# Expert 0's transposed x: built on TensorE with 0/1 choices instead of scattered and read back

## What is computed

```python
# attention: q, k, v of (2, 8, 576, 64)
scores = scale * q @ k.T
kth    = the 32nd largest score of each row
scores = where(scores >= kth, scores, -1e9)
x      = softmax(scores) @ v            # then (1152, 512): one row per token

# mixture of 8 experts with one choice per token, at most 288 tokens each
logits = x @ w_gate
e      = argmax(logits);  gate_w = softmax(logits)[e]
pos    = how many earlier tokens chose the same expert
disp[e, pos] = x                        # if pos < 288, else dropped
y      = relu(disp @ w1[e]) @ w2[e]
x      = gate_w * y[e, pos]             # 0 for a dropped token

# a last layer
h = x @ w_in                            # 2048 wide
g = (a0 + a1 h + a2 h^2 + a3 h^3) / (1 + |b0||h| + |b1| h^2 + 1e-6)
out = g @ w_out
```

## Time and profile before

| what | us |
|---|---|
| median of 3 runs | 807.46 (806.16 to 808.84) |
| the profiled execution | 809.16 |
| its span, first to last instruction | 807.4 |
| PE busy | 740.2 (92%) |
| DVE busy | 658.3 (82%) |
| ACT busy | 491.8 (61%) |
| POOL busy | 359.7 (45%) |
| mean granted PE clock | 0.958 |

### The profile page before, as it was taken

The page is one execution under the profiler, slowest core; times in us unless marked ns, Lnnn a source line. Parts: engine busy times, 40 slices in busy tenths (PEclk is TensorE's granted clock), DMA queues, the critical chain, the costliest instruction groups (busy, mean ns, idle before and its releaser), DMA issues.

```text
span 807.4 us, 15534 instructions
## 1 busy us (share of the span) xinstructions
PE 740.2 (92%) x5370; PEld 692.8 (86%) x5370; DVE 658.3 (82%) x1664; ACT 491.8 (61%) x890; POOL 359.7 (45%) x531
## 2 busy tenths in 40 slices
PE   4899999999999999838999999999469999999997
PEld 4788899898898888728999999999469899898996
DVE  3999999999999999825767667675749988898885
ACT  6677676666677775434445444544547767767673
POOL 4646565545568784240000000000149678667764
PEclk9799999999999999967999999999769999999999
DMA  9640000600000202031657677586811002000001
GB/s 190 159 163 14 1 16 1 222 15 2 14 2 15 106 7 100 1 144 44 219 173 237 194 207 238 170 210 190 230 48 31 1 1 80 1 0 19 22 1 39
DMA packets 61978, 71.20 MB, mean 88 GB/s; under 512 B 21969, under 2 KB 41937, under 8 KB 61906
## 3 DMA queue, kind: packets, MB, share of 16 engines
q1 hardware_dynamic: 60466, 65.57, 27.5%
q0 software_dynamic: 1440, 4.72, 1.7%
HBM read 56.12 MB, written 14.16 MB: 87 GB/s over the span
## 4 chain that ended last, share of the span: by engine, by line
PE 58%; DVE 26%; DMA 5%; issue 4%; ACT 3%; POOL 2%; SPq 1%; DVEq 0%; ACTq 0%; POOLq 0%
PE bank L1400 16%; PE bank L1401 16%; PE bank L1402 16%; DVE best L739 8%; DVE pairs L741 5%; DVE best L760 3%; PE bank L1306 3%; DVE pairs L758 2%; PE bank L1282 2%; PE bank L1272 2%; DMA slots_out<-y_blocks 2%; DVE pairs L722 2%; DMA slot_rows<-slots_in 2%; DVE joined L769 1%; DVE least_kept L778 1%
## 5 line engine op out<-in xcount | busy, mean ns | idle before, releaser
L957 DVE RECIPROCAL r<-c 128x384 f32<-128x384 f32 x48 | 122.5, 2552 | 25.3 <-POOL c L678 25.2
L739 DVE MAX8 best<-pairs 128x8 f32<-128x288 f32 x288 | 130.9, 547 | 0.0
L1028 ACT ACTIVATE probsT<-bank 96x768 f32<-96x768 f32 x72 | 58.2, 808 | 95.5 <-PE bank L1289 95.5
L667 POOL DMA_INDIRECT x_rows<-slots_out,slot_index x9 | 11.2, 1240 | 225.8 <-DMA slots_out<-y_blocks 224.3
L1306 PE MATMUL bank<-v_rows,probsT 96*128 96x65 f32 (+1 forms) x960 | 106.5, 264 | 3.6 <-ACT probsT L1028 3.4
L741 DVE MATCH_REPLACE8 pairs<-best,pairs 128x288 f32<-128x288 f32 x216 | 109.7, 547 | 0.0
L1306 PEld LDWEIGHTS bank<-v_rows,probsT 96*128 96x128 f32 (+1 forms) x960 | 102.3, 181 | 8.0 <-ACT probsT L1028 6.8
L886 DVE TENSOR_TENSOR wl<-raw,wh 128x1024 fp32r<-128x1024 f32 x72 | 87.2, 1218 | 19.6 <-ACT wh L1122 19.2
L1136 ACT ACTIVATE hTh<-bank 128x288 fp32r<-128x288 f32 x64 | 26.5, 414 | 104.4 <-PE bank L1402 104.4
L1400 PE MATMUL bank<-xTh,wh 128*128 128x288 f32 x256 | 76.7, 300 | 12.9 <-DVE xTl L898 12.9
L577 POOL TENSOR_TENSOR pairs<-scores 128x288 int32<-128x288 int32 x72 | 57.7, 801 | 66.3 <-ACT scores L1014 65.9
(11 more groups left out here) (138 smaller groups left out, 2201.6 us busy)
## 6 DMA issues: line engine op xcount, KB each, us to landing
raw<-in_moe_w SPq DMA_DIRECT2D x16, 2048.0 KB, 8.9
slots_in<-zeros SPq DMA_DIRECT2D x18, 256.0 KB
slot_rows<-slots_in SPq DMA_DIRECT2D x32, 144.0 KB, 8.7
slots_out<-y_blocks SPq DMA_DIRECT2D x32, 144.0 KB, 8.2
raw<-in_moe_w_in SPq DMA_DIRECT2D x8, 512.0 KB, 8.0
v_rows<-in_v SPq DMA_DIRECT2D x16, 144.0 KB, 4.0
out_rows<-out_rows SPq DMA_DIRECT2D x9, 256.0 KB, 2.4
q_rows<-in_q SPq DMA_DIRECT2D x8, 256.0 KB, 3.1
```

Source lines behind the costliest of these rows:

```text
L739: ins = nc.vector.max(best, cur)
L957: nc.vector.reciprocal(rS[x][:], cS[x][:]).then_inc(s_d2, 1)
L1028: nc.scalar.activation(pT[x % 2][:], T_ps[0:KP, 0:KJ * P], ACT.Exp, scale=SCALE).then_inc(s_ex, 1)
```

## The change

Expert 0 gets its transposed x from PE. For each tile t, DVE makes `chosen[t]`, a 128x288 matrix of 0 and 1: row = token of the tile, column = slot of expert 0, 1 where the token has that slot (`choice`). x times gate weight is written as a high part by ACT (`x_high_part`) and a low part by DVE (`low`); PE sums x_hi[t]^T chosen[t] + x_lo[t]^T chosen[t] over the nine tiles in four banks, one for each 128 columns of x (`first_x`): 72 products in all. ACT and DVE take xTh and xTl of expert 0 out of these banks. The other experts still go through DRAM: all nine tiles are scattered, and now POOL itself multiplies x by the gate weight in place before each scatter (`gated`). The read and the turn of expert 0's rows are gone. w1[0] is loaded in four DMAs in the permuted order.

Beside that: the last head is turned in banks 0 and 1 (`turned`), so its turn doesn't wait for the exponential of the head before; `times_v` of the last three heads comes after both turns. The counts of earlier tokens of a whole tile are summed by DVE in three shifted additions (`oh2`, `oh4`, `ohb`), and PE needs two products where it had eight. The routing of tile 8 reads its logits straight from the bank.

The core of the diff, PE, POOL, SP and ACT:

```diff
+        def turned(x):
+            return S_ps if x == NH - 1 else T_ps
...
-            sp.wait_ge(s_sd, 16 * NT)
-            load_rows(0)
+            sp.wait_ge(s_sd[0], 16 * FIRST_OUT)
+            sp.wait_ge(s_sd[1], 16 * (NT - FIRST_OUT))
             def expert(e, first, last):
                 if not last:
-                    sp.wait_ge(s_xt, (e + 1) * DC)
+                    if not first:
+                        sp.wait_ge(s_xt, e * DC)
                     load_rows(e + 1)
...
+            def gated(t):
+                pool.wait_ge(s_xi, t + 1)
+                pool.wait_ge(s_xo, X0_ORDER.index(t) + 1)
+                x_ = xa[:, t * DM:(t + 1) * DM]
+                nc.gpsimd.tensor_scalar(x_, x_, gw[:, t:t + 1], None, ALU.mult).then_inc(s_xg, 1)
             for i, tiles in enumerate(GATED):
                 pool.wait_ge(s_ix, i + 1)
                 for t in tiles:
+                    gated(t)
                     pool.wait_ge(s_xg, t + 1)
                     nc.gpsimd.indirect_dma_start(
...
-            for i in range(NH + 1):
+            for i in range(NH):
                 slot(i)
+            short_of(NH - 2)
+            short_of(NH - 1)
             gate_exp(0)
-            slot(NH + 1)
-            gated(0)
+            exps(NH - 2)
+            exps(NH - 1)
+            act.wait_ge(s_gw, 1)
+            for t in range(LAST - 1):
+                x_high_part(t)
             x_turned(LAST)
-            logits_out(LAST)
+            x_high_part(LAST - 1)
             gate_exp(1)
-            gated(1)
+            act.wait_ge(s_gw, 2)
+            x_high_part(LAST)
...
+                    if first and f == 0:
+                        act.wait_ge(s_sd[0], 16 * FIRST_OUT)
                     nc.scalar.activation(hTh[f % 2][:], bank(f % 2)[:, 0:CAP], ACT.Relu).then_inc(s_hh, 1)
...
+            def first_x(t, ds):
+                n_ = min((t + 1) * P, CAP) if t else CAP
+                pe.wait_ge(s_ch, CHOICES.index(t) + 1)
+                for part in range(2):
+                    if part == 0:
+                        pe.wait_ge(s_xi, t + 1)
+                    else:
+                        pe.wait_ge(s_xo, X0_ORDER.index(t) + 1)
+                    for d in ds:
+                        if t == X0_ORDER[0] and part == 0 and d >= 2:
+                            pe.wait_ge(s_xn, LAST + d - 1)
+                        ends = t == X0_ORDER[-1] and part == 1
+                        last = nc.tensor.matmul(bank(X0_BANK[d])[:, 0:n_], (x_hi, x_lo)[part][t][:, d * P:(d + 1) * P],
+                                                chosen[t][:, 0:n_], start=(t == X0_ORDER[0] and part == 0), stop=ends)
...
-            for i in range(NH + 2):
+            for i in range(NH):
                 slot(i)
+            for x in (NH - 2, NH - 1):
+                turn_scores(x)
+                less_max(x)
+                drop(x)
             tokens_before_most()
-            times_v(NH - 1)
+            for x in (NH - 3, NH - 2, NH - 1):
+                times_v(x)
+            first_x(0, range(DC - 1))
             turn_x(LAST)
+            first_x(0, range(DC - 1, DC))
+            first_x(1, range(DC))
             logits(LAST)
+            for t in X0_ORDER[2:4]:
+                first_x(t, range(DC))
             tokens_before_last()
+            for t in X0_ORDER[4:]:
+                first_x(t, range(DC))
```

and DVE after the one-hots of tiles 0 to 7:

```diff
+            def choice(t):
+                if t == 0:
+                    dve.wait_ge(s_no, 1)
+                nc.vector.tensor_scalar(chosen[t][:], slot_no[:], c0[:, t:t + 1], oh[:, t * E:t * E + 1].bitcast(F32),
+                                        ALU.is_equal, ALU.mult).then_inc(s_ch, 1)
+            def low(t):
+                dve.wait_ge(s_xi, t + 1)
+                nc.vector.scalar_tensor_tensor(x_lo[t][:], xa[:, t * DM:(t + 1) * DM], gw[:, t:t + 1],
+                                               x_hi[t][:].bitcast(F32), ALU.mult, ALU.subtract).then_inc(s_xo, 1)
...
+            gate_weights(0)
+            last_x(0)
+            before_in_first(0)
+            slot_numbers(0)
+            for t in range(3):
+                choice(t)
+                low(t)
+            last_x(1)
+            for t in (3, 4):
+                choice(t)
+                low(t)
...
+            choice(5)
+            low(5)
+            gate_weights(1)
+            before_in_first(1)
+            choice(LAST)
+            choice(6)
+            low(6)
+            low(LAST)
+            choice(7)
+            low(7)
+            slot_numbers(1)
```

More of the change, by code:

```diff
@@ L812, in link @@
                 dve.wait_ge(s_gc, chain[0])
[L814 to L852, removed]
             def last_x(half):
@@ L870, in last_x, with by_e @@
                 ins.then_inc(s_xn, 1)
[L872 to L880, removed]
+            def by_e(t, part):
+                lo, n_ = GATED[part][0], len(GATED[part])
+                return t[:, lo * E:(lo + n_) * E].rearrange("p (t e) -> p t e", t=n_)
@@ new lines, in _ @@
+            dve.wait_ge(s_sum0, 3)
+            dve.wait_ge(s_oh, 1)
+            W = LAST * E
+            link(nc.vector.tensor_tensor(oh2[:, 2 * E:2 * E + W], ohz[:, E:E + W].bitcast(F32), ohz[:, 0:W].bitcast(F32), ALU.add))
+            link(nc.vector.tensor_tensor(oh4[:, 5 * E:5 * E + W], oh2[:, 2 * E:2 * E + W], oh2[:, 0:W], ALU.add))
+            with nc.allow_low_precision("counts are whole numbers"):
+                nc.vector.tensor_tensor(ohb[:], oh4[:, 4 * E:4 * E + NT * E], oh4[:, 0:NT * E], ALU.add).then_inc(s_os, 1)
@@ L901, in _ @@
             for d in range(DC):
-                x_turned(0, d)
-            for d in range(DC):
-                x_low(0, 0, d)
+                dve.wait_ge(s_xh, d + 1)
+                nc.vector.tensor_tensor(xTl[0][:, d, :], bank(X0_BANK[d])[:, 0:CAP], xTh[0][:, d, :].bitcast(F32),
+                                        ALU.subtract).then_inc(s_xl, 1)
+            dve.wait_ge(s_ab, 32)
+            nc.vector.tensor_scalar(ab[:, 6:8], ab[:, 4:6], -1.0, None, ALU.mult).then_inc(s_ab, 1)
+            dve.wait_ge(s_ab, 33)
+            nc.vector.tensor_tensor(ab[:, 6:8], ab[:, 6:8], ab[:, 4:6], ALU.max).then_inc(s_ab, 1)
             def y_out(e):
@@ L1095, in _, with x_high_part @@
             k_out(3, 1)
[L1096 to L1101, removed]
+            def x_high_part(t):
+                if t == LAST:
+                    act.wait_ge(s_fx, 1)
+                nc.scalar.activation(x_hi[t][:], xa[:, t * DM:(t + 1) * DM], ACT.Copy, scale=gw[:, t:t + 1]).then_inc(s_xi, 1)
             def gate_exp(part):
@@ L1288, in drop @@
                 for j in range(KJ):
-                    last = nc.tensor.matmul(T_ps[0:KP, j * P:(j + 1) * P], so[x % 2][:, j * KP:(j + 1) * KP], minus_big[:],
+                    last = nc.tensor.matmul(turned(x)[0:KP, j * P:(j + 1) * P], so[x % 2][:, j * KP:(j + 1) * KP], minus_big[:],
                                             start=False, stop=(j in (3, KJ - 1)), skip_group_check=True)
@@ L1329, in tokens_before_most @@
             def tokens_before_most():
-                pe.wait_ge(s_oh, 1)
+                pe.wait_ge(s_os, 1)
                 pe.wait_ge(s_const, 4)
[L1333 to L1339, removed]
@@ L1346, in tokens_before_last @@
                 pe.wait_ge(s_oh, 2)
[L1347 to L1348 removed]
+                nc.tensor.matmul(bank(COUNTS)[:, LAST * E:NT * E], tri[:], oh[:, LAST * E:NT * E], start=False, stop=True,
+                                 skip_group_check=True).then_inc(s_po, 1)
+            def first_x(t, ds):
[12 more added lines that the diff above has]
+                                                chosen[t][:, 0:n_], start=(t == X0_ORDER[0] and part == 0), stop=ends)
+                        if ends:
+                            last.then_inc(s_x0, 1)
+                if t == 0 and DC - 1 in ds:
+                    last.then_inc(s_fx, 1)
```

114 lines of the change are left out of this document (92 added, 22 removed).

## The result

The changed kernel takes 812.24 us (median of 6 runs, 811.04 to 813.44) against 808.04 us for the kernel before in the same set of runs (6 runs, 806.16 to 809.34): ratio 1.0056, 95% interval 1.0041 to 1.0071. It is slower by 4.2 us, where 7 us less were forecast. The profiled execution took 812.47 us with a span of 810.7.

What follows compares the result with a forecast made beforehand. PE, busy 92% of the span, bounds: 6.7 us from expert 0's earlier start, 2.3 from full clock, less 1.0 for expert 1's rows and 1.0 for a clock fall, gain 7.0, from 807.46 to 800.5 us; range 796.5 to 804.5.

Steps and rivals of the forecast that it cites:

- What bounds, and the new order: Before expert 0: PE bounds; PE makes x^T itself instead of waiting for scatter and read; start 360.0 instead of 366.70.
- DVE's choice: On DVE before expert 0: 128x288, once per tile, taken at 0.36 us, bounds 0.2 and 0.43.
- low part: On DVE before expert 0: 128x512, once per tile, taken at 0.62 us, bounds 0.55 and 0.75.
- What is late next: Expert 1's rows, behind POOL's multiplies and scatters, arrive at 372.9; w2_step(3) of expert 0 starts at 373.8, costing 1.0 us.
- The multiply: POOL's gate multiplication, once per tile before its scatter: taken at 1.3 us, between 0.578 and 1.39.
- The handover from the multiply to the issue: On POOL, between each tile's multiply and its scatter: 0.16 us.
- The issue itself: POOL's issue of each tile's scatter, an indirect DMA: 1.04 us.
- The clock after the pause: PE in expert 0, after waiting for expert 1's rows: a clock fall costs up to 2.1 us, taken as 1.0.
- rival 1: POOL's multiply is cheap (0.98 us) and expert 1's rows come in time: gain 9.0 to 11.0, 797.5 us; chance 0.22.
- Rival 2: PE stays at half clock from 346.8 until expert 0: gain 0 to 2.1, time 806.4 us; chance 0.13.
- Rival 3: DVE's low parts hold up POOL's multiplies; slower from 3.4 us a tile, 813.3 at a 2.6 us multiply; chance 0.06.

Runs made afterwards that it cites:

- The experiment with the shifted scatter: Changed kernel with the multiply of tile t + 1 ahead of the scatter of tile t on POOL: 806.77 us, ratio 0.9976 to the kernel before.

## Why the prediction was wrong

**What bounds, and the new order: held, the digits by luck.** The start of expert 0, S, was forecast at 360.0 and measured at 359.99, at full clock as forecast. But the attention ended 1.4 us earlier in this profile (POOL's last max parts at 334.23 against 335.68), which lies within the spread of executions given above; counted from there S took 25.8 us, where my count has 24.3. Of the 1.4 more, 0.9 lie between the last tile's turn and expert 0 (14.1 us against 13.2), with the clock fallen as forecast. PE was the longer engine there, as forecast. DVE's choice (0.42 long) and low part (0.75 long) stood at the upper ends of their bounds, and beside a multiply on POOL beyond them (0.71 and 0.80 for the choice, 1.17 for the low part).

**What is late next: the right wait, at a wrong price. This is the step that failed.** The prediction put the wait for the rows of expert 1 at f = 2 of expert 0, with hTl(3) behind it, and its relation between the rows' arrival R and PE's next product, start = R + 0.88, holds to the digit: 383.18 + 0.88 = 384.06. The end of the last issue, T, was forecast at 366.8 and came at 377.05, R at 383.2 instead of 372.9; PE's pause was 11.0 us instead of 1.0. By term:
- The multiply: 1.3 forecast, 1.77 on average over the nine (1.58 undisturbed), 4.3 us in all. My upper bound, 1.39, was a straight line through two small forms; the true price lies above it, and above the two-tensor form of the same size (1.279). One input was no reason for a lower price.
- The handover from the multiply to the issue: 0.16 forecast, 0.82 measured, 5.9 us in all and the largest part. The row I took it from had an indirect DMA that waited for nothing of POOL's; this one waits for the instruction in front of it. The experiment with the shifted scatter shows just this difference, 0.80 against 0.17. The prediction had no bounds for this term.
- The issue itself: 1.04 forecast, 1.18 measured, 1.2 us.
These are 11.4 us; 1.2 less, since the first multiply started at 342.83 instead of 344.0: 10.3 us.

**The clock after the pause**: 1.0 forecast. The 11 us cost a full fall, 16 products at 0.24 us in 384:388, 1.9 us. So the account closes: 7.0 forecast, less 10.3 for T, less 0.9 for the clock, is 4.2 slower, and 4.2 were measured between the medians. That these digits meet is partly luck. The two profiles the account is made from differ by 3.3 us in their spans; at the first product of the last layer the changed kernel is still 4.0 behind (591.28 against 587.28), the 0.7 are made up after it, and nothing here shows by what. And without the attention's early end this profile would have been some 1.4 us longer.

**The rivals.** The condition of rival 1, a cheap multiply, is refuted. What it would bring if the rows came in time is right: 797.5 forecast, 795.4 to 801.5 with the multiplication off POOL. The estimate of 0.95 us from the Trainium skill (GPSIMD Engine Reference, 3.1 Elementwise) does not fit either: this operation, with a scalar per partition, takes 1.58. Rival 2 is out: the clock was back before expert 0. Rival 3 gave nearly the measured outcome (813.3), and its place; its point of decision was a tile of 3.4 us, and tiles took 3.8. Its mechanism was the smaller part of it: disturbed multiplies and issues add 1.7 and 1.3 us, 3 of the 10.3. And my argument against it, that DVE has nothing left after 356 to hold POOL up, was wrong: the slowest multiply, 2.49, started at 365.42, beside expert 0's 128x1024 subtract, which itself took 1.63 (at 364.85) instead of 1.23. I gave rival 3 a chance of 0.06. It needed a tile to be only a third dearer than a sum of a multiply that no row showed and a handover read from another situation, so that was too little.

**The range** carried bounds for the multiply, too low at their upper end, and none for the handover, for which I had taken a single value from one row.

## What to carry to other kernels

When a critical transfer is taken off the path, price the next user of the same path as carefully as the first: here the rows of the second expert were wanted 9 us after the first expert's start, and nine multiplications and nine handovers were added in front of them. Where POOL's line of indirect DMAs is what others wait for, put no elementwise operation into it; put it on an engine that is idle in that stretch, and if it has to stay, place another POOL instruction between it and the DMA that waits for it. Moving the consumer later inside a loop cost time in every pass here (0.5 us an expert), and gained only once. And take a price from a row in which the instruction waits for the same thing as in the new kernel.

## What the hardware showed unexpectedly

- On POOL, 128x512 float32 times a scalar per partition takes 1.58 us, more than a two-tensor subtraction of that size (1.279).
- An indirect DMA that waits for the POOL instruction just ahead of it starts 0.80 us after the end of that one. If it waits for the instruction before the last, it starts 0.17 us after the end of the last; directly behind another indirect DMA, 0.30.
- Side by side POOL's multiply and DVE's operations on SBUF take longer, now the one, now the other: the first multiply took 2.16 us beside a low part of 0.75. Here is a low part (it reads two SBUF tensors) of the changed kernel, where the multiply of 347.26 to 348.87 runs beside it, and one of the kernel without multiplications. The Trainium skill (GPSIMD Engine Reference, 8. Key points) says that the two contend for SBUF when DVE reads two SBUF inputs; these rows agree with it.
```profile
347.36 1.17 DVE L914 SCALAR_TENSOR_TENSOR x_low<-x_all,gate_weight,x_high 128x512 fp32r<-128x512 f32 x1
```
```profile
345.48 0.75 DVE L905 SCALAR_TENSOR_TENSOR x_low<-x_all,gate_weight,x_high 128x512 fp32r<-128x512 f32 x1
```
- The clock before expert 0 fell in one execution of a kernel and not in another, once beginning in a window in which PE was busy throughout (342:344 above, 0.91), and in three profiles it stayed up over a gap of 1.73 us. It is worth 3.5 us. A gap of 1.5 us is thus no sure sign of a fall, as I had taken it.
